# Down product of two expert layers: the residual of the down weights kept in 4 bytes, and one 512-column matmul for two products

## The reference, cut to what matters

```python
h = np.maximum(x[mask] @ w1[e], 0.0)          # w1[e]: 256 x 1024
out[mask] = gate_w[mask, None] * (h @ w2[e])  # w2[e]: 1024 x 256
```

## Time and profile before

| | us |
|---|---|
| median of 2 runs | 3052.76 (3051.33 to 3054.19) |
| profiled execution, span from first to last instruction | 3076.1 |
| PE busy | 2812.8 |
| PE weight loads busy | 2407.7 |
| DVE busy | 1899.2 |
| ACT busy | 1035.3 |
| POOL busy | 639.3 |
| mean granted TensorE clock | 0.960 |

### The profile page before, as it was taken

The page is one execution under the profiler, slowest core; times in us unless marked ns, Lnnn a source line. Parts: engine busy times, 40 slices in busy tenths (PEclk is TensorE's granted clock), DMA queues, the critical chain, the costliest instruction groups (busy, mean ns, idle before and its releaser), DMA issues. The chain is left out here.

```text
span 3076.1 us, 81536 instructions
## 1 busy us (share of the span) xinstructions
PE 2812.8 (91%) x22933; PEld 2407.7 (78%) x22934; DVE 1899.2 (62%) x7285; ACT 1035.3 (34%) x2269; POOL 639.3 (21%) x620
## 2 busy tenths in 40 slices
PE   5777662899999999999999959999999999999998
PEld 4666552788888888888888848888888888888886
DVE  8887883588988989898898963232323232232322
ACT  3444542233333333333333313333333332333332
POOL 0455354011111111111111111111111111111111
PEclk9788886899999999999999989999999999999999
DMA  8466444333333332323232251222211211221210
GB/s 270 160 221 221 150 166 139 142 105 113 113 109 110 110 130 86 133 64 135 90 108 91 66 187 49 83 69 98 89 61 48 99 47 42 85 83 43 87 41 21
DMA packets 194629, 327.71 MB, mean 107 GB/s; under 512 B 21652, under 2 KB 137633, under 8 KB 188066
## 3 DMA queue, kind: packets, MB, share of 16 engines
q1 hardware_dynamic: 165474, 250.25, 25.4%
q0 software_dynamic: 28992, 75.94, 7.0%
HBM read 779.66 MB, written 135.23 MB: 297 GB/s over the span
## 5 line engine op out<-in xcount | busy, mean ns | idle before, releaser
L1160 PE MATMUL m_hbank<-m_xT_high,up_high 128*128 128x256 f32 x3296 | 1178.2, 365 | 7.1 <-DVE m_xT_low L956 6.9
L967 DVE SCALAR_TENSOR_TENSOR m_hT_low<-m_hbank,m_hT_high 128x512 bf16<-128x512 f32 x824 | 567.8, 689 | 997.1 <-ACT m_hT_high L1084 971.7
L1181 PE MATMUL m_ybank<-ring_high,m_hT_high 128*128 x3296 | 1178.1, 363 | 1.5 <-issue 1.5
L1182 PE MATMUL m_ybank<-ring_high,m_hT_low 128*128 x3296 | 945.9, 287 | 0.0
L1161 PE MATMUL m_hbank<-m_xT_low,up_high 128*128 128x256 bf16 x3296 | 938.4, 285 | 0.0
L1162 PE MATMUL m_hbank<-m_xT_high,up_low 128*128 128x256 bf16 x3296 | 915.1, 278 | 0.0
L1183 PE MATMUL m_ybank<-ring_low,m_hT_high 128*128 x3296 | 891.6, 270 | 0.0
L1084 ACT ACTIVATE m_hT_high<-m_hbank 128x512 fp32r<-128x512 f32 x824 | 490.2, 598 | 660.0 <-PE m_hbank L1162 654.4
L1160 PEld LDWEIGHTS m_hbank<-m_xT_high,up_high 128*128 128x128 f32 x3296 | 627.8, 190 | 62.0 <-issue 14.7
L1181 PEld LDWEIGHTS m_ybank<-ring_high,m_hT_high 128*128 128x128 f32 x3296 | 619.6, 188 | 54.3 <-issue 1.9
L979 DVE SCALAR_TENSOR_TENSOR m_product<-m_yr,m_gates 128x256 f32<-128x256 f32 x1648 | 598.6, 419 | 0.6 <-ACT m_yr L1115 0.6
(11 more groups left out here) (186 smaller groups left out, 2240.9 us busy)
## 6 DMA issues: line engine op xcount, KB each, us to landing
ring_high<-w_high SPq DMA_DIRECT2D x212, 1024.0 KB, 8.3
up_high<-w_high SPq DMA_DIRECT2D x208, 1024.0 KB
ring_low<-w_low SPq DMA_DIRECT2D x212, 512.0 KB, 9.1
up_low<-w_low SPq DMA_DIRECT2D x208, 512.0 KB
m_xt<-records SPq DMA_DIRECT2D x208, 258.0 KB, 2.7
m_raw<-in_weights SPq DMA_DIRECT2D x24, 698.0 KB, 5.7
w_high<-m_high SPq DMA_DIRECT2D x24, 698.0 KB, 3.3
raw<-in_weights SPq DMA_DIRECT2D x64, 256.0 KB
```

Source lines behind the costliest of these rows:

```text
L967: nc.vector.scalar_tensor_tensor(hT_low[:, j % 2, 2 * i:2 * i + 2, :], hbank[i][:].rearrange("p (c t) -> p c t", c=2), 0.0, hT_high[:, j % ...
L1160: nc.tensor.matmul(h, w, high, start=(c == 0), stop=False)
L1181: nc.tensor.matmul(y, high, ring_high[:, cols], start=(c == 0), stop=False)
L1182: nc.tensor.matmul(y, low, top_half(ring_high[:, cols]), start=False, stop=False)
```

## The change

The residuals of all weights are kept in 4 bytes instead of 2, in the DRAM tensor `w_low` and in SBUF; the up product reads the upper half of it. The rings of the down weights become one tensor, so that 256 columns of `high` and the 256 of `low` form one moving operand of 512 columns. In `down` the triple becomes a pair: `low` block times the top half of the high weights (256 columns, bf16), and `high` block times both (512 columns, float32r). The second 256 columns of the bank thus gather the residual's product; each half s has a bank of its own. ScalarE scales the first half of the bank as before, and now increments `y_half`; a new function `join` on VectorE adds the gate times the second half to `yr` and increments `y_scaled`. `join` of tile j is the last thing in VectorE's order for tile j, in both layers.

```diff
-    w_low = nc.dram_tensor("w_low", (P, 2 * E, WCOLS), bf16).ap()
+    w_low = nc.dram_tensor("w_low", (P, 2 * E, WCOLS), f32).ap()
...
-        up_low = sb("up_low", [P, 2, W2], bf16)
+        up_low = sb("up_low", [P, 2, W2], f32)
...
-            low = [sb(f"low{i}", [P, WCH], bf16, sa) for i in range(DEPTH)]
+            low = [sb(f"low{i}", [P, WCH], f32r, sa) for i in range(DEPTH)]
...
-        ring_high = sb("ring_high", [P, RING * W2], f32r)
-        ring_low = sb("ring_low", [P, RING * W2], bf16)
+        ring = sb("ring", [P, 2, RING * W2], f32r)
+        ring_high, ring_low = ring[:, 0, :], ring[:, 1, :]
...
-                    low = sb(name + "low", [P, SPLIT], bf16, sm)
+                    low = sb(name + "low", [P, SPLIT], f32r, sm)
...
-                ybank = pb(name + "ybank", [P, 512], f32, sm)
+                ybank = [pb(name + f"ybank{s}", [P, 512], f32, sm) for s in range(2)]
...
+                    def join(g, j):
+                        dve.wait_ge(y_half, g * 4 + (j + 1))
+                        for s in range(2):
+                            y = nc.vector.scalar_tensor_tensor(yr[:, j, s, 0:DIM], ybank[s][:, DIM:2 * DIM], meta[:, j, s, 0:1],
+                                                               yr[:, j, s, 0:DIM], ALU.mult, ALU.add)
+                        y.then_inc(y_scaled, 1)
...
                                 nc.vector.tensor_copy(idx[:, j, :], meta[:, j, :, 1]).then_inc(route2, 1)
+                            join(g, j)
...
-                                y = nc.scalar.activation(yr[:, j, s, 0:DIM], ybank[:, s * DIM:(s + 1) * DIM], ACT.Copy,
+                                y = nc.scalar.activation(yr[:, j, s, 0:DIM], ybank[s][:, 0:DIM], ACT.Copy,
                                                          scale=meta[:, j, s, 0:1])
-                            y.then_inc(y_scaled, 1)
+                            y.then_inc(y_half, 1)
...
-                                    w, w_rest = up_high[:, j % 2, at:at + P], up_low[:, j % 2, at:at + P]
+                                    w, w_rest = up_high[:, j % 2, at:at + P], top_half(up_low[:, j % 2, at:at + P])
...
-                            y = ybank[:, s * DIM:(s + 1) * DIM]
-                            nc.tensor.matmul(y, high, ring_high[:, cols], start=(c == 0), stop=False)
-                            nc.tensor.matmul(y, low, top_half(ring_high[:, cols]), start=False, stop=False)
-                            last = nc.tensor.matmul(y, top_half(high), ring_low[:, cols], start=False, stop=(c == FC - 1))
+                            y = ybank[s][:, 0:DIM]
+                            nc.tensor.matmul(y, low, top_half(ring_high[:, cols]), start=(c == 0), stop=False, skip_group_check=True)
+                            last = nc.tensor.matmul(ybank[s][:], high, ring[:, :, cols], start=False, stop=(c == FC - 1),
+                                                    skip_group_check=True)
```

More of the change, by code:

```diff
@@ L227, in first_down @@
             sp.dma_start(ring_high[:, place].bitcast(f32), w_high[:, layer * E + e, W2:WCOLS]).then_inc(w_first[layer][e], 16)
-            sp.dma_start(ring_low[:, place], w_low[:, layer * E + e, W2:WCOLS]).then_inc(w_first[layer][e], 16)
+            sp.dma_start(ring_low[:, place].bitcast(f32), w_low[:, layer * E + e, W2:WCOLS]).then_inc(w_first[layer][e], 16)
         with ExitStack() as sa:
@@ L340, in split_pieces @@
                             at = b * (QP * WCH) + n * WCH
-                            for dst, src in ((flat_high, high[buf][:].bitcast(f32)), (flat_low, low[buf][:])):
+                            for dst, src in ((flat_high, high[buf][:].bitcast(f32)), (flat_low, low[buf][:].bitcast(f32))):
                                 out_ = dst[:, at:at + WCH] if isinstance(b, int) else dst[:, bass.ds(at, WCH)]
@@ L887, in load_down @@
                         to = bass.ds(field(t, NEXTSLOT, (RING - 1) * W2), W2)
[L888 removed]
+                        for ring, src in ((ring_high[:, to].bitcast(f32), w_high), (ring_low[:, to].bitcast(f32), w_low)):
                             sp.dma_start(ring, src[:, bass.ds(nxt + m * E, 1), W2:WCOLS].rearrange("p e n -> p (e n)"),
@@ L915, in body @@
                             sp.dma_start(flat_high[:, bass.ds(at + LAYER, SPLIT)], high[:].bitcast(f32)).then_inc(split_stored, 16)
-                            sp.dma_start(flat_low[:, bass.ds(at + LAYER, SPLIT)], low[:]).then_inc(split_stored, 16)
+                            sp.dma_start(flat_low[:, bass.ds(at + LAYER, SPLIT)], low[:].bitcast(f32)).then_inc(split_stored, 16)
                     groups(sp, body)
```

2 lines of the change are left out of this document (1 added, 1 removed).

## The result

The changed kernel takes 3090.99 us, median of 2 runs (3089.35 and 3092.63), against 3052.76 before: ratio 1.0129, 95% interval 1.0109 to 1.0149. It is slower by 38 us, where the forecast was 3047 and the range ended at 3085. Its profiled execution has a span of 3087.5 us and a time of its own of 3089.35. The profiled execution of before, 3076.1, stands 23 us above its runs; its layer 0 begins at 546.3 us. The stages are therefore set against another profile of the same kernel (`before_again`, span 3050.0, layer 0 from 519.4), in which the other stages are as long within 1 us. Only layer 0's third interval differs, 12.0 and 16.0 us.

What follows compares the result with a forecast made beforehand. TensorE's pace was taken to bound both layers, VectorE close behind in layer 0. Terms -16.5 + 0 + 0.8 + 5 + 3.5 + 1.5 = -5.7 us took 3052.8 to 3047 us; range for 8 in 10: 3005 to 3085.

Steps and rivals of the forecast that it cites:

- Term 2: `join` on VectorE in layer 0: 0.68 us a tile fits VectorE's room, cost 0; at the kernel's end +0.8 us.
- Rival 2: VectorE becomes layer 0's bound, `join` waiting for ScalarE's scaling: layer 0 loses 98 us, 3154 us in all; chance 0.07.
- point of decision: Layer 0: VectorE becomes the bound once `join` costs over 0.97 us a tile, 0.68 + 0.29.
- Term 1: Down product's pair instead of triple: 5 ns gained per pair, 16.5 us in all; bounds a loss and 36 ns.
- Terms 3 and 4: Doubled residual bytes: +5 us in the transform, +3.5 between the layers, +1.5 at layer 0's start.
- Transform: Each batch of the transform stores 1 MB more: +5 us, bounds 0 and 23.
- Between the layers: 1.5 MB more loaded ahead of the padding stores delays layer 1's first load: +3.5 us, bounds 0 and 4.
- At the end: At the kernel's end `join` stands between scaling and last store: +0.8 us.
- Layer 0's start: 2 MB more ahead of the conditional load of tile 2's up weights: +1.5 us, bounds 0 and 3.
- Expert reloads: Loads for a new expert grow from 1.5 to 2 MB where DMA engines are a third busy: 0.
- The up product's step of two: `up` reads its residual with a step of two, as L1161's weights are read already: 0.

Runs made afterwards that it cites:

- join_only: Kernel before plus `join` on VectorE with constant factor 0.0; triples, bytes and rings as before: 3104.88 us, ratio 1.0042 to before.
- no_join: Changed kernel without `join`, the second 256 columns computed but not added: 3099.36 us, ratio 1.0024 to before.
- turn_halved: Changed kernel with VectorE's loop body written twice, so it turns after 8 tiles instead of 4: 3067.28 us, ratio 1.0063 to before.
- two_of_256: Changed kernel with the pair's 512-column matmul written as two of 256 columns with the same 4-byte block: 3118.47 us.
- no_low: Changed kernel without the down product's bf16 matmul, leaving the 512-column matmul and its load: 2991.50 us.
- bytes_only: Kernel before with all residuals in 4 bytes and the two-part ring, three matmuls as before, no `join`: 3109.90 us, ratio 1.0059 to before.
- gates_early: Changed kernel with the next layer's gates loaded ahead of the down weights of experts 1 to 3: 3083.98 us, ratio 1.0118 to before.

## Why the prediction was wrong, step by step

**Term 2, `join` in layer 0, is the step that failed: "Room is left, 0.29 us a tile."** Its price was nearly right, 0.80 us of VectorE for a forecast of 0.68 from L979 (the row with the constant factor; `join_only`, with such a factor, adds 0.66 to 0.70 a pass). The pass without it was right as well: 10.46 us at its shortest for 10.56. The mean was wrong. It had three of the four kinds of pass in it and left out the one with the turn: 2.24 us of gap in the mean, 0.56 a tile. The forecast's own 4 x 11.64, with this gap and 4 x 0.12 for the dearer `join`, is 49.3 us a group; 49.2 was measured, against 48.2 of TensorE: VectorE needs 0.26 us a tile more than TensorE, where the forecast had it at 0.29 less. Some 22 us are this: 22.4 by `no_join` (3121.75 - 3099.36), 22.9 by `turn_halved` in layer 0.

The rows for it stood in the trace of before. The tile of the earlier trace rows was one without a turn, and of the idle time before L967 (90.8 us in 800 to 1700) 74.2 had the name of ScalarE's relu and 16.6 of "issue". Read one tile earlier, the relu was through 2.30 us before its reader began, and 2.48 in the mean of the turns: about half of the 90.8 us was not a wait. The 0.70 us of the earlier trace rows, at a tile without a turn, was one, and `join` did fill it.

**Rival 2** had the right mechanism with 0.07 and was priced from a wait for ScalarE that never came: 3154. Its point of decision, 0.97 us a tile, lacks the turn; with it, it is (48.2 - 4 x 10.46 - 1.5 - 2.5) / 4 = 0.59, and `join` costs 0.80. Its sign in the trace, idle of TensorE on `m_xT_low` in layer 0 above 5 us, came (26.9 of the 28.5 us are there), but it was set too low to tell: before has 6.9 us of it.

**Term 1, the pair: forecast 5 ns gained a step, measured 3 ns lost** (0.359 against 0.356 to 0.357), within the bounds of -10 to 36. The reading behind the term, that a 4-byte load is just not covered by 256 columns, did not stand: by it `two_of_256` should have cost 50 ns or more, and it cost 3 to 4. Nor does a load come free: 19 ns stay beyond the columns of each of the two matmuls (`no_low`). The chosen value was near the seam of 3 ns between two matmuls, which the removal of a matmul did not win. The formula of 2.5 ns for each matmul that the prediction quotes from the Trainium skill would have given a gain too. Layer 1 is still 1.8 us shorter, by a path for which the forecast has no term: TensorE's turn no longer costs 0.25 us a group, which outweighs the slower steps. So of the 16.5 us forecast none came the way it was argued, which is the second part of the error.

**Terms 3 and 4.** Transform +9.0 for 5, in its bounds; on other chips 0 to 5. Between the layers +3.3 for 3.5, which is right in this pair of profiles and partly luck: in the eleven profiles with bytes and `join` together this stretch is 57.1 to 60.6 us against 54.2 to 54.5 before, so +3 to +6, and the one term is made of two. `no_join` and `bytes_only` have 56.7 (+2.4, the bytes), `join_only` 56.0 (+1.7, `join`, for which the forecast put nothing there). At the end +1.8 for 0.8, and +3.3 (42.1 us) in `gates_early` and `turn_halved`. Layer 0's start: +3.4 for 1.5, or +7.5 against the other two profiles of before, whose third interval was 12.0 and 11.9; above its bound of 3, and by another transfer than the one argued from; the forecast looked at the up load of tile 2 and not at all that stands behind the enlarged loads in SyncE's order. Expert reloads 0: no tile after the third waits for them. The up product's step of two 0: a triple of `up` takes 0.357 us in the median before and 0.357 to 0.358 after.

The stages add up to 9.0 + 25.2 + 3.3 - 1.8 + 1.8 = 37.5 us. That is the difference of the two profiled spans and cannot be otherwise; the result is 38.2. The prediction took 2% as what a measurement can tell from no change; the intervals of the runs are 0.1 to 0.2% to either side, so the 1.3% are clear of noise.

## What to carry to other kernels

Before an engine that is 88% busy is given more work, add up a whole period of its loop, the turn included, and not the pass that is easiest to read: the room is the period of the bounding engine less this sum. A long idle time in front of one line is only room as far as the instruction it waits for really ends late; compare the two times. An instruction taken out of the bounding engine is worth its columns first: here a matmul less in every step, with the columns kept, saved no time in the step and 0.25 us at the turn of the loop. Put every transfer queued behind a load that grows on the list, the broadcast constants too. With the gates early and VectorE's turn halved the changed kernel is level with before, not ahead of it.

## What the runs showed of the hardware

- A turn of VectorE's loop of 359 to 367 recorded instructions costs 2.0 to 2.9 us in after and ended 1.2 to 1.8 us after an 8 KB transfer of instructions had landed, in every version looked at; written twice as long, it costs the same half as often. In `no_low` it cost 5.5 to 7.2 us.
- A turn of TensorE's loop costs 0.25 us at 993 recorded instructions, nothing at 833 or, doubled, at 1578, 2.4 to 4.2 at 1664 (once 9.3) and 5 to 7 at 1897 to 1987 (three times 8 to 9). Doubling VectorE's body gave 23 us; with ScalarE's and TensorE's doubled too, the kernel before lost 129 us.
- A GpSimd subtraction of 3.2 us held a VectorE instruction with two SBUF inputs for 0.96 us in the mean, one with an input in PSUM not at all.
- Two scalar_tensor_tensor of 256 columns take 0.87 us with a factor from SBUF (after) and 0.75 with a constant (`join_only`).
- 768 columns took 0.357 to 0.363 us as two or three matmuls with one or two 4-byte blocks.
